# GpSimd takes all inversion rounds but the first, ScalarE issues the y stores, and the loads and double product steps are laid out anew

## The reference

```python
k_n = k / (np.linalg.norm(k, axis=-1, keepdims=True) + 1e-06)      # 4 batches, 8 heads, 768 tokens, 48 dims
for t in range(S):
    kt, vt, bt = (k_n[:, :, t], v[:, :, t], beta[:, :, t, None])
    y[:, :, t] = np.einsum('bhd,bhde->bhe', q[:, :, t], state)
    v_old = np.einsum('bhde,bhd->bhe', state, kt)
    state = state + bt[:, :, :, None] * np.einsum('bhd,bhe->bhde', kt, vt - v_old)
...
h = x @ w_in                                                       # 3072 x 384 by 384 x 2048
g = P / (Q + 1e-06)                                                # rational in h; second layer: relu(h)^2
return (g @ w_out).astype(np.float32)
```

## Time and profile before

| | us |
|---|---|
| median of 3 runs | 1160.2 (1158.51 to 1162.98) |
| the profiled execution | 1163.1 |
| its span | 1161.4 |
| attention part, to the first instruction of the feed-forward part | 353.07 |
| start_z(0) | 54.45 |
| TensorE busy | 1108.2 |
| VectorE busy | 714.1 |
| ScalarE busy | 655.0 |
| GpSimd busy | 454.3 |

### The profile page before, as it was taken

The page is one execution under the profiler, slowest core; times in us unless marked ns, Lnnn a source line. Parts: engine busy times, 40 slices in busy tenths (PEclk is TensorE's granted clock), DMA queues, the critical chain, the costliest instruction groups (busy, mean ns, idle before and its releaser), DMA issues.

```text
span 1161.4 us, 18190 instructions
## 1 busy us (share of the span) xinstructions
PE 1108.2 (95%) x6356; PEld 954.9 (82%) x6356; DVE 714.1 (61%) x1228; ACT 655.0 (56%) x1309; POOL 454.3 (39%) x519
## 2 busy tenths in 40 slices
PE   8779878999996999999999999899999999999998
PEld 6579878999995878888888888788888888888886
DVE  6777773773337998888787888856333333334332
ACT  5536554754448978777777878745333333333332
POOL 5184075028104977777777777700000000000000
PEclk8989898999997999999999999999999999999999
DMA  9926765665434101010100103042010101010000
GB/s 201 207 44 140 134 147 102 142 123 93 95 103 142 56 1 55 1 55 1 33 23 1 55 1 109 14 134 71 1 55 1 55 1 55 1 55 1 1 28 28
DMA packets 173626, 74.41 MB, mean 64 GB/s; under 512 B 135968, under 2 KB 161696, under 8 KB 172576
## 3 DMA queue, kind: packets, MB, share of 16 engines
q1 hardware_dynamic: 173536, 73.26, 26.4%
HBM read 52.27 MB, written 20.71 MB: 63 GB/s over the span
## 4 chain that ended last, share of the span: by engine, by line
PE 64%; DVE 3%; ACT 1%; issue 1%; ACTq 0%; DVEq 0%
PE ps_y L1126 11%; PE ps_h L1111 11%; PE ps_y L1128 11%; PE ps_y L1127 11%; PE ps_h L1113 11%; PE ps_h L1112 11%; DVE w_in_lo L1245 1%; DVE g_hi L1275 1%; DVE cubic L1260 1%; DVE ps_h L1282 0%; DVE w_out_lo L1248 0%; DVE g_lo L1290 0%; DVE ps_h L1266 0%; ACT w_in_hi L1149 0%; ACT coef L1169 0%
## 5 line engine op out<-in xcount | busy, mean ns | idle before, releaser
L1111 PE MATMUL ps_h<-x_hi,w_in_lo 128*128 128x512 f32 x576 | 227.0, 394 | 13.6 <-DVE g_lo L1290 6.9
L1113 PE MATMUL ps_h<-x_hi,w_in_hi 128*128 128x512 f32 x576 | 226.3, 393 | 0.0
L1112 PE MATMUL ps_h<-x_lo,w_in_hi 128*128 128x512 f32 x576 | 226.3, 393 | 0.0
L1126 PE MATMUL ps_y<-g_hi,w_out_lo 128*128 128x512 f32 x576 | 224.6, 390 | 0.1
L1127 PE MATMUL ps_y<-g_lo,w_out_hi 128*128 128x512 f32 x576 | 224.3, 389 | 0.0
L1128 PE MATMUL ps_y<-g_hi,w_out_hi 128*128 128x512 f32 x576 | 224.1, 389 | 0.0
L1301 DVE TENSOR_TENSOR q<-h_sq 128x512 f32<-128x512 f32 x96 | 66.4, 692 | 135.4 <-ACT h_sq L1190 133.8
L1197 ACT ACTIVATE g_hi<-q 128x512 fp32r<-128x512 f32 x96 | 60.9, 634 | 141.6 <-PE ps_y L1128 137.1
L1111 PEld LDWEIGHTS ps_h<-x_hi,w_in_lo 128*128 128x128 f32 x576 | 109.3, 190 | 38.0 <-DVE g_lo L1290 8.1
L1113 PEld LDWEIGHTS ps_h<-x_hi,w_in_hi 128*128 128x128 f32 x576 | 109.4, 190 | 23.2
L1370 POOL TENSOR_TENSOR head_times_q<-q,g_hi 128x512 f32<-128x512 f32 x96 | 124.2, 1294 | 10.7 <-DVE g_hi L1275 10.7
(11 more groups left out here) (101 smaller groups left out, 1980.6 us busy)
## 6 DMA issues: line engine op xcount, KB each, us to landing
kq<-kq_in SPq DMA_DIRECT2D x10, 768.0 KB, 5.6
shared<-w_in SPq DMA_DIRECT2D x32, 192.0 KB, 4.1
shared<-w_out SPq DMA_DIRECT2D x32, 192.0 KB, 4.3
vkp<-k_in SPq DMA_DIRECT2D x12, 384.0 KB, 5.1
vkp<-v_in SPq DMA_DIRECT2D x12, 384.0 KB, 5.4
iq<-kq_in SPq DMA_DIRECT2D x12, 384.0 KB, 4.5
x_first<-y_t SPq DMA_DIRECT2D x24, 192.0 KB, 2.7
shared<-x_first SPq DMA_DIRECT2D x6, 768.0 KB, 5.8
```

The lines of the kernel that those rows point to most:

```text
L1111: pe.matmul(bank(n), lo, x_hi[:, slot, k, :], start=(k == 0), stop=False)
L1112: pe.matmul(bank(n), hi, x_lo[:, slot, k, :], start=False, stop=False)
L1113: mm = pe.matmul(bank(n), hi, x_hi[:, slot, k, :], start=False, stop=(k == KT - 1))
L1126: pe.matmul(ps_y[m][:, :], lo, g_hi[:, d, :], start=(f == 0), stop=False)
```

## The change

- Rounds 1 to 5 of the inversion are GpSimd's, one after the other, each followed by `scale_v` of its two quads. VectorE keeps round 0.
- ScalarE issues `store_y`, in odd steps from 3 on.
- Two product groups in steps 2 to 6, one in step 1 and in steps 7 to 27.
- Quad 1 is placed by both engines: two slices by ScalarE in step 1, and one by VectorE in each of steps 1 and 3. Square sums, `scale_v` on VectorE and `store_n` move to other steps.
- On SP `store_inverse` goes ahead of `load_blocks`, `load_inverse` (which also waits for `z_done` of the step before the slot's reuse) ahead of `load_cross` and of that step's loads of K, kq and V; `load_kq(7)` moves from step 5 to step 6.
- 13 later warm-up matmuls for 20. SP waits for all y stores at the end of the attention part.

```diff
-    TWICE = 6
-    LEAD = UPFRONT + TWICE - 1
+    TWICE = (2, 6)
+    LEAD = UPFRONT + TWICE[1] - TWICE[0]
...
-    BY_POOL = (1, 3, 5)
-    INV_FROM = {2: 7, 4: 21}
-    INV_TO = (None, 6, 15, 21, 29, 37)
+    INV_OUT = (None, 6, 14, 21, 28, 36)
     V_BY_DVE = (1, 2)
-    WARM_FIRST, WARM_LATER = 14, 20
+    WARM_FIRST, WARM_LATER = 14, 13
...
         def square_step(h):
-            return 2 * (h - 5) if h < 8 else 4 * h - 25
+            return 2 * h - 9 if h < 7 else 4 * h - 22
...
             def load_inverse(h):
 
                 sp.wait_ge(inv_stored, 16 * (h // 2))
+                sp.wait_ge(z_done, 4 * h - 4)
...
+                for r in range(1, ROUNDS):
+                    if n == INV_OUT[r]:
+                        store_inverse(r)
                 for r in range(2, ROUNDS):
                     if n == max(8 * r - 12, 6):
                         load_blocks(r)
-                if n >= 4 and n % 2 == 0:
-                    store_y((n - 4) // 2)
+                for h in range(2, QUADS):
+                    if n == max(4 * h - 3, INV_OUT[h // 2]):
+                        load_inverse(h)
+                        load_cross(h)
...
                 for h in range(6, QUADS):
-                    if n == ({6: 3, 7: 5}[h] if h < 8 else 4 * h - 25):
+                    if n == ({6: 4, 7: 6}[h] if h < 8 else 4 * h - 24):
                         load_kq(h)
...
             for i in range(2):
-                sp.wait_ge(y_stored[i], 16 * (GROUPS // 4 - 1))
+                sp.wait_ge(y_stored[i], 16 * (GROUPS // 4))
...
-            for h in (3, 4, 5):
-                scale_v(h)
-            invert(3, 0, INV_OPS)
-            for h in (6, 7, 8, 9):
-                scale_v(h)
-            invert(5, 0, INV_OPS)
-            for h in (10, 11):
-                scale_v(h)
+            scale_v(3)
+            for r in range(2, ROUNDS):
+                invert(r)
+                scale_v(2 * r)
+                scale_v(2 * r + 1)
...
+                if n >= 3 and n % 2 == 1:
+                    store_y((n - 3) // 2)
...
-                if n in (1, 2):
-                    for s in (2 * n - 2, 2 * n - 1):
-                        place_quad(1, s)
+                if n in (1, 3):
+                    place_quad(1, 2 + n // 2)
...
                 for h in V_BY_DVE:
-                    if n == 2 * h:
+                    if n == 2 * h + 1:
                         scale_v(h)
```

More of the change, by code:

```diff
@@ L52, in mid_group @@
     def mid_group(n):
-        return UPFRONT + 2 * (n - 1) if 1 <= n <= TWICE else None
+        return UPFRONT + 2 * n - TWICE[0] - 1 if TWICE[0] <= n <= TWICE[1] else None
     def end_group(n):
[L58 to L62, removed]
+        if mid_group(n) is not None:
+            return mid_group(n) + 1
+        if n < TWICE[0]:
+            return UPFRONT + n - 1 if n > 0 else None
+        return n + LEAD if n < GROUPS - LEAD else None
+    DVE_N = tuple(range(FIRST)) + tuple(mid_group(n) for n in range(TWICE[0], TWICE[1] + 1))
     ACT_N = tuple(g for g in range(GROUPS) if g not in DVE_N)
@@ L350, in _ @@
                         load_v(h)
[L351 to L357, removed]
                 if n == GROUPS - 6:
@@ L360, in _, with invert @@
                     moe_inputs.load_first(sp, x_out)
-            store_y(GROUPS // 2 - 1)
             for i in range(2):
-                sp.wait_ge(y_stored[i], 16 * (GROUPS // 4 - 1))
+                sp.wait_ge(y_stored[i], 16 * (GROUPS // 4))
         @block.gpsimd
         def _(pool):
-            def invert(r, first, last):
+            def invert(r):
                 x = inv[:, r % INV_RING]
-                for i in range(first, last):
-                    j, done = i // 2, (INV_OPS - 1) * (r // 2) + i
+                for i in range(INV_OPS):
+                    j, done = i // 2, (INV_OPS - 1) * (r - 1) + i
                     if i == 0:
@@ L714, in _ @@
                     roots(norm_chunk(4))
-                if 2 <= n < TWICE:
+                if n == 1:
+                    for s in range(2):
+                        act.activation(*place(1, s), ACT.Copy).then_inc(placed_by_act, 1)
+                if TWICE[0] <= n < TWICE[1]:
                     spread_keys(8 + n)
-                if n >= TWICE and n % 2 == 0 and end_group(n + 1) is not None:
+                if n > TWICE[1] and n % 2 == 1 and end_group(n + 1) is not None:
                     spread_keys((n + 1 + LEAD) // 2)
+                if n >= 3 and n % 2 == 1:
+                    store_y((n - 3) // 2)
                 for h in range(5, QUADS):
@@ L803, in take_products, with invert_first @@
                                   before[:, :].unsqueeze(1).to_broadcast([P, PAIRS, C]), ALU.mult).then_inc(p_ready, 1)
[L805 to L809 removed]
+            def invert_first():
+                x = inv[:, 0]
+                for i in range(INV_OPS):
+                    j, done = i // 2, i
                     if i == 0:
[L811 to L814 removed]
+                        dve.wait_ge(blocks_turned, 1)
                         dve.tensor_tensor(x, x, upper[:, :, :], ALU.mult).then_inc(dve_inv_step, 1)
@@ L830, in invert @@
                         step = dve.tensor_tensor(rest, rest, part, ALU.add)
-                        step.then_inc(inv_ready[r] if i == INV_OPS - 1 else dve_inv_step, 1)
+                        step.then_inc(inv_ready[0] if i == INV_OPS - 1 else dve_inv_step, 1)
             def effective_q(n):
@@ L893, in _ @@
                     take_products(end_group(n - 1))
-                for r in INV_FROM:
-                    if INV_FROM[r] <= n < INV_TO[r]:
-                        now, end = inverted(r, n), inverted(r, n + 1)
-                        invert(r, now, max(end - 2, now))
                 if mid_group(n) is not None:
@@ L902, in _ @@
                     effective_q(n - 1)
-                for r in INV_FROM:
-                    if INV_FROM[r] <= n < INV_TO[r]:
-                        now, end = inverted(r, n), inverted(r, n + 1)
-                        invert(r, max(end - 2, now), end)
                 if n < GROUPS:
```

34 lines of the change are left out of this document (12 added, 22 removed).

## The result

The changed kernel takes 1331.68 us (median of 4 executions, 1329.88 to 1333.08) where the kernel before takes 1161.22 (4 executions, 1158.51 to 1162.98): a ratio of 1.147 [1.144, 1.150]. The forecast of 1146 has the wrong sign. The profiled execution took 1333.08 us, with a span of 1331.4.

The account below looks back on a forecast made before the run. TensorE was taken to bound the attention part, apart from waits in steps 0 to 7, 15 and 16. Terms -1.4, -6.0, -13.1, +0.9, +2.0, +2.2 sum to -15.4, giving 1147.7 or 1144.8: forecast 1146 us, range 1136 to 1154.

Parts of the forecast that it names:

- The step that failed: Opening claim on the second part, from 353.07 us on: the change does not touch it.
- Start: Warm-up before step 0: start_z(0) 2.4 us earlier, 1.0 given back to low clock; term -1.4, from -2.4 to +0.6.
- Steps 0 to 8: Early attention steps: changed VectorE order shortens waits, two new waits appear; term -6.0 us (-8.4 to -3.1).
- scale_v(1): New wait at start_z(4): TensorE waits 3.8 us for VectorE's scale_v(1), then 2.8 more from slow clock.
- kq: New wait in step 7: ScalarE stands 2.2 to 4.7 us for load_kq(7), queued behind loads of the inverse.
- Steps 9 to 16: With round 2 on GpSimd, the 10.0 us inverse wait before step 16 and its slow clock go; term -13.1 us.
- the margin of 4 us: Slack for round 2 on GpSimd: step 16's loads there by 104.5, the step beginning at 108.3 us after start_z(0).
- Step 27: One product group moves into this step; term +0.9 us.
- Step 40: Round 5 on GpSimd is tight, so TensorE may wait for its inverses; term +2.0 us (0 to +6).
- Handover: Between the parts: SP waits for all y stores, so the second part starts after the last lands; term +2.2 us.
- Stores on ScalarE: Issuing y stores from ScalarE fits its gaps of some 1.2 us a step, so it costs nothing.
- rival C: ScalarE's 24 stores at 2.41 us each would hold z_first(n+1) and make the kernel slower, 1174 us; chance 3%.

Follow-up runs that it names:

- e1: The changed kernel with the table-set preload moved from step 21 to step 23, behind the last square root: 1156.18 us, ratio 0.994.
- e2: The kernel before with only the table-set preload moved from step 21 to step 19, ahead of its last square root: 1337.77 us, ratio 1.151.
- e3: The changed kernel with a second table-set preload at the head of ScalarE's feed-forward part: 1154.98 us, ratio 0.993.
- e5: e1 with SP waiting at the end of the attention part for all but the last y stores, as before: 1146.62 us; same program again 1149.54.
- e4: e1 with 20 later warm-up matmuls again instead of 13: 1158.56 us, ratio 0.997.
- e14: e12 with 20 later warm-up matmuls instead of 13: 1152.38 us, ratio 0.991.
- e6: e1 with scale_v(1) in VectorE's step 2 and load_kq(7) back in step 5: 1150.93 us, ratio 0.990.
- e10: e1 with scale_v(1) in VectorE's step 2 and nothing else: 1152.52 us, ratio 0.994.
- e12: e11 with GpSimd waiting for VectorE's scales of quad 6 before its eight masks: 1147.53 us, ratio 0.987.
- e7: e6 with SP not waiting for the last two y stores and 20 later warm-up matmuls: 1151.94 us, ratio 0.991.
- e9: e1 with the y stores issued by SP again, at their place before the change: 1155.66 us, ratio 0.994.
- e11: e10 with SP not waiting for the last two y stores and load_kq(7) issued between load_blocks(2) and load_inverse(2): 1147.01 us, ratio 0.990.

## Why the prediction was wrong

**The step that failed** stands at the head of the prediction: "The second part, from 353.07 us on, is not touched." Its lines are not; what it takes over from the first is. The change was then taken part by part, and `square_step` was followed on VectorE (as scales(5) and sums(6)) and not on ScalarE, where the new formula moves `roots(11)` by three steps past an instruction placed by a number of its own. No rival had it. It costs 172 us in the second part, the whole of the loss and a little more; e1, e2 and e3 each show it.

With the tables repaired (e1: -0.6%, some 7 us; forecast -15.4):

- **Start**, -1.4: right for start_z(0), not for the clock. start_z(0) came at 52.0 to 53.5 in the traces of all other kernels with 13 warm-up matmuls, and at 55.30 in that of the changed kernel, where the last placement ended only at 55.15. The price of the low clock, 1.0 (0 to 3), was too small: it came to 4.4 us by step 4 in e1, and to nothing in e5. By the medians e4 and e14 put the cut at 2 to 5 us, not clear of the noise.
- **Steps 0 to 8**, -6.0: the term that failed beside the tables. Step 9 came at t 77.5 (e1: 78.1) where 65.1 to 70.4 was forecast and 73.5 is the kernel before. Played through, step 4 was to start at 27.5, step 6 at 44.7 and step 7 at 51.4; e5 has 27.2, 44.3 and 51.0, and its step 9 at 69.6. So the path was right for an execution without half clock at the start in which scales(6) does not meet GpSimd's masks. Two pieces were mis-sized. Steps 0 to 3 took 32.4 us in the changed kernel and 31.6 in e1, with the half clock. Step 5 was put at 7.5 us (37.2 to 44.7) and took 13.4 in the changed kernel, 11.2 in e1 and 7.1 in e5: in the changed kernel the nine operations of scales(6) took 5.12 us, TensorE waited 3.4 for the mask behind them, and 6.8 us of half clock followed at 103.3. At 0.57 us each these operations lie inside the "0.4 to 1.0 us each" of the prediction; what it had at nothing in step 5 was the wait behind them and the slow clock after it. The kernel before has the same scales at 89.03, ahead of its masks at 92.6. The forecast named the contention and looked for it only in the length of GpSimd's rounds. The Trainium skill (SBUF — State Buffer, Who interferes with whom) states that a VectorE instruction with two SBUF inputs contends with GpSimd's reads, and that one with a single input, outside the two-port modes, does not; the rows of L748 and L744 agree.
- **scale_v(1)**: 3.8 us of wait forecast, 3.8 measured (3.6 to 3.9 in e1, e4, e5). **kq**: 2.2 to 4.7 forecast, 4.3 measured in the changed kernel, 5.8 in e1 and 6.0 in e5. That the changed kernel's lies in the range is in part luck: the inverse's store landed after 3.8 us, near the 3.0 of the good end, and kq took 7.5 from issue to landing for the 5.6. That taking both away brings little (e6, e10) was not foreseen: the loads of the inverse are next in line at nearly the same time.
- **Steps 9 to 16**, -13.1: 47.1 us for the forecast 46.1, so -12.1. The wait of 10.0 us before step 16 is gone, but the margin of 4 us was not there: start_z(16) waits 0.7 us for the last load of its quad in the changed kernel and 1.1 to 3.0 in every repaired trace but e12's (2.2 in e1, 3.0 in e10). From the store of round 2 to its last load's landing were to be 9.3 to 11.8 us and are 16.9 (157.12 to 174.00): the store alone takes 8.0 to land, issued right behind a load of kq. The prediction had 3.0 to 5.5 for it, a median and the shortest; the kernel before already has 7.0 for the one at 167.69.
- **Step 27**, +0.9: it lasts 5.8 for 4.9, as said (by the earlier trace rows the products would be 1.0, 5.83 less 4.82). **Step 40**, +2.0: no wait in the changed kernel and e1 (1.2 and 1.0 us in e4 and e7); steps 28 to 39 took 57.8. Steps 17 to 27 took 65.1 where 61.8 and 0.9 were forecast: steps 20, 22 and 24 last 6.4, 6.4 and 6.8 for 5.8. The table load at 209.85 lies in step 22; in e1, where it doesn't, steps 17 to 27 take 63.6. Step 24 has the root's load in it (222.08), with a wait of 0.5 us for z_first behind, and in e1, where it lasts 6.6, the preload (220.59). In step 20 two operations of scales(10) take 1.38 and 1.45 us on VectorE beside two scale_v of GpSimd, the overlap of step 5 again.
- **Handover**, +2.2: 2.85 us from the last store's issue to the second part for 0.89, so +2.0; in the trace of e5 it is 0.81 again.
- **Stores on ScalarE**, nothing: right (e9), and rival C fell with it.

## What to carry to other kernels

An engine carries state across a program: the table set in ScalarE, as much as a buffer. Where a change moves any instruction that needs another set (here one square root a quad), look where the last of them now stands against every placed load, and count the loads in the trace before anything else. Where a cover for TensorE's clock is cut, price the low clock by the instructions that would run in it: here 4.4 us over 193 of them. Where two engines' chains pass close by each other, compare the same line's operations in two executions: small ones with two SBUF inputs show the overlap first. Taking away a wait pays only to where the next thing in line stands: e6 took away two waits of 3.9 and 5.8 us for some 5 in all, e10 one of 3.9 for nothing that can be measured.

The best version measured is e12 (the table set behind the last root, scale_v(1) in step 2, load_kq(7) in the gap, the short handover, the masks behind the scales): 1147.53 us, ratio 0.987 [0.985, 0.989], below the kernel before and the changed one. It is not clear of e5, e6 or e11, whose intervals touch its own.

## What the runs showed of the hardware

- A table load takes 1283 ns each of 192 times, and ScalarE's busy time rises by 247.1 us, 1.287 for each: no time beyond the load itself is seen.
- Of 247 us more on ScalarE, 172 show in the time: 75 were gaps of ScalarE behind TensorE (its wait for the first layer's h_sq falls from 76.4 us to 1.1). TensorE's own busy time in that part rose from 791 to 835 us with a granted clock of 0.96 for 0.99: 86.6 us of half clock in 16 stretches, for 21.1 in 4 in e1. It now waits 68 times for g_lo; that these waits bring the low clock is argued, not shown apart.
- The low clock of the earlier trace rows begins at 70.8, inside the wait that ends at 72.00, and not only behind it.
- A store of an inverse takes 3.8 us to land at 109.39 and 8.0 at 157.12, where a load of kq was issued 0.5 us before it.
- SP's issue of one load is not a constant. In the changed kernel, with four loads of inverses just issued, K and kq took 2.05 and 2.67 us where the forecast put 0.48 on each:

```profile
116.75 2.05 SPq L213 DMA_DIRECT2D vkp<-k_in  x1
118.84 2.67 SPq L226 DMA_DIRECT2D kq<-kq_in  x1
```
